# An attention, routed experts and FFN kernel: the opening of the attention reordered, and products of ones in TensorE's waits

## The reference

```python
# q, k, v: (4, 12, 448, 64)
scores = matmul(q, k.T) / sqrt(64) - log(448)
x = matmul(sigmoid(scores), v)            # tokens (1792, 768)

logits = x @ w_gate                       # (1792, 8)
# (token, expert) pairs in falling order of logit; a pair is taken where the
# token is free and the expert has under 224 tokens
out[mask_e] = relu(x[mask_e] @ w1[e]) @ w2[e]      # for the 8 experts e, F = 1024

h = x @ w_in                              # (768, 2048)
out = (max(h, 0) + alpha * min(h, 0)) @ w_out
```

## Time and profile before

| | |
|---|---|
| median of 3 runs | 1068.9 us (1068.49 to 1069.94) |
| profiled execution, its time | 1074.37 us |
| profiled execution, its span | 1072.7 us |
| mean granted clock | 0.964 |
| TensorE busy | 978.1 us, 91% |
| VectorE busy | 588.4 us, 55% |
| ScalarE busy | 393.0 us, 37% |
| HBM traffic | 206 GB/s over the span |

### The profile page before, as it was taken

How to read it: one execution, slowest core, us unless ns; L and a number is a source line. 1 busy time by engine, 2 the same in 40 slices (tenths; PEclk the granted TensorE clock), 3 DMA queues, 4 the chain that set the end, 5 groups by cost and what they waited for, 6 DMA issues and landing times.

```text
span 1072.7 us, 16546 instructions
## 1 busy us (share of the span) xinstructions
PE 978.1 (91%) x6340; PEld 841.6 (78%) x6340; DVE 588.4 (55%) x1454; ACT 393.0 (37%) x628; POOL 185.5 (17%) x202
## 2 busy tenths in 40 slices
PE   5999999806969999799999999999999999999994
PEld 3555555406969898699989998998899999989993
DVE  2344444597765836966954586497539637211110
ACT  4676777401042123346312224542222355122212
POOL 0010110105150010233301014350100325100001
PEclk9999999956979999999999999999999999999997
DMA  9799997317379586847777855679685446966501
GB/s 213 204 260 270 275 264 228 135 35 236 103 206 363 191 221 181 285 128 223 265 280 235 239 177 130 190 222 368 208 241 195 151 129 188 375 231 220 177 1 51
DMA packets 121476, 222.32 MB, mean 207 GB/s; under 512 B 51424, under 2 KB 69216, under 8 KB 121408
## 3 DMA queue, kind: packets, MB, share of 16 engines
q1 hardware_dynamic: 88064, 120.34, 35.7%
q0 software_dynamic: 21280, 91.59, 27.4%
q10 hardware_dynamic: 12064, 9.47, 3.4%
HBM read 184.84 MB, written 36.52 MB: 206 GB/s over the span
## 4 chain that ended last, share of the span: by engine, by line
PE 83%; DVE 10%; ACT 2%; DMA 1%; issue 1%; POOL 0%; SPq 0%; ACTq 0%; DVEq 0%; POOLq 0%
PE psum L886 19%; PE psum L874 19%; PE psum L821 11%; PE psum L851 11%; PE psum L633 7%; PE psum L617 7%; DVE hits L1348 4%; PE psum L816 2%; PE psum L601 2%; PE psum L846 2%; PE psum L644 1%; DVE unit L1243 1%; DMA stage<-x_rows,tok_idx 1%; PE psum L768 1%; PE psum L652 1%
## 5 line engine op out<-in xcount | busy, mean ns | idle before, releaser
L886 PE MATMUL psum<-g_high,unit 128*128 128x448 f32 x768 | 231.7, 369 | 6.4 <-DVE g_low L1271 6.2
L874 PE MATMUL psum<-y_high,unit 128*128 128x448 f32 x768 | 231.5, 369 | 4.6 <-ACT below L1021 4.3
L886 PEld LDWEIGHTS psum<-g_high,unit 128*128 128x128 f32 x768 | 144.3, 188 | 21.8 <-DVE g_low L1271 9.9
L874 PEld LDWEIGHTS psum<-y_high,unit 128*128 128x128 f32 x768 | 144.3, 188 | 18.8 <-ACT below L1021 5.8
L874 PE MATMUL psum<-y_low,unit 128*128 128x448 f32 x384 | 140.5, 366 | 0.0
L886 PE MATMUL psum<-g_low,unit 128*128 128x448 f32 x384 | 140.5, 366 | 0.0
L1243 DVE TENSOR_TENSOR unit<-raw,unit 128x768 fp32r<-128x768 f32 (+1 forms) x106 | 109.3, 1060 | 39.7 <-ACT unit L994 39.2
L1020 ACT ACTIVATE above<-psum 128x448 f32<-128x448 f32 x64 | 35.0, 546 | 246.2 <-PE psum L874 246.2
L821 PE MATMUL psum<-x_high,unit 128*128 128x224 f32 x672 | 119.8, 280 | 2.9 <-DVE unit L1243 2.9
L1266 DVE SCALAR_TENSOR_TENSOR below<-below,neg_alpha,above 128x448 f32<-128x448 f32 x64 | 43.8, 684 | 138.1 <-ACT below L1021 137.7
L851 PE MATMUL psum<-h_high,unit 128*128 128x224 f32 x672 | 117.2, 278 | 2.5 <-issue 2.5
(11 more groups left out here) (159 smaller groups left out, 1278.7 us busy)
## 6 DMA issues: line engine op xcount, KB each, us to landing
unit<-ffn_parts SPq DMA_DIRECT2D x120, 768.0 KB, 6.4
ffn_parts<-pre_parts POOLq DMA_DIRECT2D x24, 768.0 KB, 5.7
ffn_parts<-unit SPq DMA_DIRECT2D x8, 768.0 KB, 5.5
q_in<-in_q_dram SPq DMA_DIRECT2D x24, 224.0 KB, 3.9
k_in<-in_k_dram SPq DMA_DIRECT2D x24, 224.0 KB, 5.9
v_in<-in_v_dram SPq DMA_DIRECT2D x24, 224.0 KB, 6.2
x_rows<-x_tok POOLq DMA_DIRECT2D x8, 672.0 KB, 5.5
rank_in<-suit_flat POOLq DMA_DIRECT2D x6, 896.0 KB, 14.2
```

The costliest lines, as they stand in the source:

```text
L874: last = pe.matmul(psum[:, IN_BANK, 0:PAIR], w, y[:, c, :], start=(c == 0 and i == 0), stop=(c == DC - 1 and i == 2))
L886: last = pe.matmul(psum[:, OUT_BANK + d, 0:PAIR], w, g[:, m % 2, :], start=(m == 0 and i == 0), stop=(m == FC - 1 and i == 2))
```

## The change

The attention's opening:

- ACT issues the first k, ahead of `w_gate` and `alpha`; SP issues the others. In the first batch SP does not wait for the semaphores that VectorE sets, and v of a pair is issued after q and k of the next pair.
- POOL's diagonal pattern has a semaphore of its own; VectorE makes `ones_f` first and `ident` next, before the other patterns. TensorE waits for `ident_done` in place of `const_done`.
- ACT does a Sigmoid of one column of ones into `counts` before it waits for `const_done`.
- TensorE does 12 products of `ones_f` with itself, then `turn_qk(0,0)`, `score(0,0,0)`, `turn_qk(0,1)`, `score(0,0,1)`. ACT does `sigmoids(0,0,0)` before the roundings of pair 1.

The routings: `keep_busy(n, bank)` issues n bf16 products of `ones_b` (112 x 112) with 448 columns of ones, into a PSUM bank that holds nothing. 120 stand after `turn_suit(0)`, 12 after `spread_thr(0)`, 18 after `sum_flags(0)`, and at step `OWN` 22 before and 12 after `turn_first(1)`.

```diff
+    FILLERS = 12
+    BUSY_SEARCH, BUSY_FLAGS, BUSY_PLACES, BUSY_TOKENS, BUSY_SPLIT = 120, 12, 18, 22, 12
...
 # SP
-            with sp.Fori(0, B) as b:
-                for hp in range(PAIRS):
-                    n = pair(b, hp)
-                    sp.wait_ge(qk_turned, turned(n - RING, 1))
-                    sp.dma_start(q_in[hp % RING][:], rows(q)).then_inc(qk_loaded[hp % RING], 16)
-                    sp.dma_start(k_in[hp % RING][:], rows(k)).then_inc(qk_loaded[hp % RING], 16)
-                    sp.wait_ge(heads_done, heads(n - V_RING))
-                    sp.dma_start(v_in[hp % V_RING][:], ...)
+            def load_qk(b, hp, first):
+                n = pair(b, hp)
+                if not first or n >= RING:
+                    sp.wait_ge(qk_turned, turned(n - RING, 1))
+                sp.dma_start(q_in[hp % RING][:], pair_rows(q, b, hp)).then_inc(qk_loaded[hp % RING], 16)
+                if not first or n > 0:
+                    sp.dma_start(k_in[hp % RING][:], pair_rows(k, b, hp)).then_inc(qk_loaded[hp % RING], 16)
+            def load_v(b, hp, first):
+                if not first:
+                    sp.wait_ge(heads_done, heads(pair(b, hp) - V_RING))
+                sp.dma_start(v_in[hp % V_RING][:], ...)
+            def load_batch(b, first):
+                for hp in range(PAIRS + 1):
+                    if hp < PAIRS:
+                        load_qk(b, hp, first)
+                    if hp > 0:
+                        load_v(b, hp - 1, first)
+            load_batch(0, True)
+            with sp.Fori(1, B) as b:
+                load_batch(b, False)
...
 # POOL
-                last.then_inc(iota_done, 1)
+                last.then_inc(diff_done if at == I_DIFF else iota_done, 1)
...
 # TensorE
-            pe.wait_ge(const_done, 1)
+            pe.wait_ge(ones_done, 1)
+            for i in range(FILLERS):
+                pe.matmul(psum[:, i % JT, 0:128], ones_f[:], ones_f[:], start=True, stop=True)
+            pe.wait_ge(ident_done, 2)
             turn_qk(0, 0)
+            score(0, 0, 0)
             turn_qk(0, 1, second=True)
-            score(0, 0, 0)
             score(0, 0, 1)
...
+            def keep_busy(n, bank):
+                for _ in range(n):
+                    pe.matmul(psum[0:P, bank, 0:4 * P], ones_b[:], ones_b[:].unsqueeze(1).to_broadcast([P, 4, P]),
+                              start=True, stop=True)
...
                 if s == OWN:
+                    keep_busy(BUSY_TOKENS, EC // 2 - 1)
                     turn_first(1)
+                    keep_busy(BUSY_SPLIT, EC // 2 - 1)
...
             turn_suit(0)
+            keep_busy(BUSY_SEARCH, Y_BANK)
             spread_thr(0)
+            keep_busy(BUSY_FLAGS, Y_BANK)
             sum_flags(0)
+            keep_busy(BUSY_PLACES, Y_BANK)
             sum_idx(0)
...
 # ACT
+            act.dma_start(k_in[0][:], first_k).then_inc(qk_loaded[0], 16)
             act.dma_start(w_gate_sb[:], w_gate.rearrange("(c p) e -> p c e", p=128)).then_inc(small_loaded, 16)
             act.dma_start(alpha_sb[:], alpha).then_inc(small_loaded, 16)
+            act.wait_ge(ones_done, 1)
+            act.activation(counts[:], ones_f[:, 0:1], ACT.Sigmoid)
             act.wait_ge(const_done, 1)
...
             for hp in range(2):
                 for i in range(2):
                     round_qk(0, hp, i, second=(hp == 1))
-            sigmoids(0, 0, 0)
+                if hp == 0:
+                    sigmoids(0, 0, 0)
...
 # DVE
+            dve.memset(ones_f[:], 1.0).then_inc(ones_done, 1)
...
-            dve.wait_ge(iota_done, len(IOTAS))
+            dve.wait_ge(diff_done, 1)
+            dve.tensor_copy(iota_f[:, I_DIFF:I_DIFF + 128], iota_i[:, I_DIFF:I_DIFF + 128]).then_inc(ident_done, 1)
+            dve.wait_ge(ident_done, 1)
+            dve.tensor_scalar(ident[:], iota_f[:, I_DIFF:I_DIFF + 128], 0.0, None, ALU.is_equal).then_inc(ident_done, 1)
+            dve.wait_ge(iota_done, len(IOTAS) - 1)
...
-            dve.tensor_scalar(ident[:], iota_f[:, I_DIFF:I_DIFF + 128], 0.0, None, ALU.is_equal)
-            dve.memset(ones_f[:], 1.0)
```

More of the change, by code:

```diff
@@ L237, in attention_routed_moe_prelu_ffn @@
         TX = RT[:, 512 - 2 * P:512]
+        ones_done = sem("ones_done")
+        diff_done = sem("diff_done")
+        ident_done = sem("ident_done")
         iota_done = sem("iota_done")
@@ L348, in probs_of, with pair_rows @@
             return PROBS0 + 4 * n + 2 * step + h + 1
+        def pair_rows(src, b, hp):
+            return src[bass.ds(b, 1), 2 * hp:2 * hp + 2].rearrange("a h (p j) d -> p j (a h) d", p=P)
+        first_k = pair_rows(k, 0, 0)
         OWN = DC + EC
@@ L431, in _ @@
         def _(sp):
-            with sp.Fori(0, B) as b:
-                for hp in range(PAIRS):
-                    def rows(src):
-                        return src[bass.ds(b, 1), 2 * hp:2 * hp + 2].rearrange("a h (p j) d -> p j (a h) d", p=P)
-                    n = pair(b, hp)
-                    sp.wait_ge(qk_turned, turned(n - RING, 1))
-                    sp.dma_start(q_in[hp % RING][:], rows(q)).then_inc(qk_loaded[hp % RING], 16)
-                    sp.dma_start(k_in[hp % RING][:], rows(k)).then_inc(qk_loaded[hp % RING], 16)
-                    sp.wait_ge(heads_done, heads(n - V_RING))
-                    sp.dma_start(v_in[hp % V_RING][:],
-                                 v[bass.ds(b, 1), 2 * hp:2 * hp + 2].rearrange("a h (p j) d -> p (a h) j d", p=P)).then_inc(v_loaded[hp % V_RING], 16)
+            def load_qk(b, hp, first):
+                n = pair(b, hp)
+                if not first or n >= RING:
+                    sp.wait_ge(qk_turned, turned(n - RING, 1))
+                sp.dma_start(q_in[hp % RING][:], pair_rows(q, b, hp)).then_inc(qk_loaded[hp % RING], 16)
[4 more added lines that the diff above has]
+                    sp.wait_ge(heads_done, heads(pair(b, hp) - V_RING))
+                sp.dma_start(v_in[hp % V_RING][:],
+                             v[bass.ds(b, 1), 2 * hp:2 * hp + 2].rearrange("a h (p j) d -> p (a h) j d", p=P)).then_inc(v_loaded[hp % V_RING], 16)
+            def load_batch(b, first):
[7 more added lines that the diff above has]
+                load_batch(b, False)
             for piece in range(PRE_ALL - PRE_RING, PRE_ALL):
@@ L1106, in _ @@
             dve.sem_inc(pre_split, PRE0)
-            dve.wait_ge(iota_done, len(IOTAS))
+            dve.wait_ge(diff_done, 1)
[3 more added lines that the diff above has]
+            dve.wait_ge(iota_done, len(IOTAS) - 1)
             for at, n, _, _, _ in IOTAS:
-                last = dve.tensor_copy(iota_f[:, at:at + n], iota_i[:, at:at + n])
+                if at != I_DIFF:
+                    last = dve.tensor_copy(iota_f[:, at:at + n], iota_i[:, at:at + n])
             last.then_inc(const_step, 1)
```

## The result

| | before | after |
|---|---|---|
| median of 16 runs each, same chip | 1070.49 us (1068.17 to 1073.77) | 1064.81 us (1062.98 to 1068.21) |
| profiled execution, its time | 1074.37 us | 1063.21 us |
| profiled execution, its span | 1072.7 us | 1061.5 us |

The ratio is 0.994, 95% interval 0.993 to 0.9951: faster by 5.7 us. I had forecast 1057.9 us in a range of 1054 to 1063.5, so the time lies outside it, and the gain is about half of the 11.0 us. Yet the two profiled executions are 11.2 us apart. Both facts need an explanation.

The account below looks back on a forecast made before the run. TensorE, busy 91% of the span, was taken as the bound, with time only in its waits and low clock. Opening 6.8 + first routing 0.8 + second expert 3.4 = 11.0 us off 1068.9 gave 1057.9 us, range 1054 to 1063.5.

Parts of the forecast that it names:

- steps 1 to 8: Attention's opening, from first q and k to `score(0,1,1)`: start at 21.5 instead of 28.3 us, 6.8 us gained.
- step 1: Opening: q and k issued at 0.9 us, both landed at 4.9; upper bound 6.3, from the second k's 5.40 us.
- the bound of 6.3: Opening: latest landing of the first k, by the 5.40 us of the second k; opening then gives 6.3 us.
- step 3: Opening: 12 products of ones at 0.25 us each, 3.0 us, from 1.1 to 4.1, hidden by q and k landing.
- steps 4 to 7: Opening: transposes at 4.9, ACT's first copy 6.8, `score(0,0,0)` at 8.55, second table load gone, `score(0,1,0)` at 17.7 not 22.54.
- Rival B: Attention is bound by DMA after all and swallows the opening's gain: 1064.7 us; 5 in 100.
- The table load: Opening: ACT's 1.28 us load moves to about 2.4 us, hidden; copy needs no third load; second load gone.
- The search's 120: First routing: 120 products from 212.5 end at 236.7 to 238.6, TensorE needed at 238.56; hidden.
- 12: 2.4 us in the 3.3 free: First routing: the 12 flags products take 2.4 us within 3.3 us free on TensorE, so hidden.
- the term of 0.8 us: First routing: high clock shortens thr, flags and the token sum by 0.3 + 0.1 + 0.4 us.
- Rival D: Products of ones too slow, search block ends some 19 to 23 us late at low level: 1080 us; 3 in 100.
- Do these pass on?: Routings: gains pass on, as queues behind depend on TensorE's progress; second expert's high clock gives 3.4 us in all.

Follow-up runs that it names:

- kernel 7: New opening without its 12 products of ones and with none in the routings, against the kernel before: 1066.52 us, ratio 0.9951.
- kernel 3: The kernel before with only `keep_busy` and its five calls in the routings, on the old opening: 1071.98 us, ratio 1.0008 to the kernel before.
- kernel 5: New opening with only the 22 and 12 products around the second expert's transposes, against the kernel before: 1065.21 us, ratio 0.9935.
- kernels 3 and 4: The second of these: the whole change with 134 search products in place of 120, against the kernel before: 1063.74 us, ratio 0.9931.

## Why the prediction was wrong, by its own steps

Starts of TensorE's work in the profiled executions, in us earlier than in the kernel before:

| start of | changed | opening alone | 22 and 12 | 22 and 12, pass moved |
|---|---|---|---|---|
| `score(0,1,1)` | 8.7 | 8.7 | 8.7 | 8.2 |
| suitability transposes | 8.8 | 8.8 | 8.7 | 8.3 |
| flags' sums | 8.0 | 9.4 | 8.9 | 7.5 |
| first expert's transposes | 8.0 | 9.5 | 9.0 | 7.4 |
| second expert | 8.8 | 8.9 | 10.3 | 7.8 |
| its second half | 11.5 | 8.5 | 13.0 | 10.5 |
| first FFN | 10.1 | 8.5 | 10.7 | 10.5 |
| second expert pair | 10.3 | 8.5 | 9.1 | 10.5 |

In the last profile the suitability transposes ran low (3.23 us for the 16 against 1.75), so its search began later; that is its smaller lead at the flags.

- **The opening, steps 1 to 8: right in mechanism, too small.** 6.8 us forecast, 8.7 us in the profiles, 8.0 us in the medians (1063.2 against 1071.2). Two sizes were off and opposed. In step 1 I took k to be there at 4.9, and wrote that nothing else is in flight; with nothing in its way the transpose waited until 6.18. SP now issues the next pairs without waiting, and of the transfers issued in the first 4 us k took 5.0 us to land in kernel 7 and 5.3 in the changed one, against 4.0 before. That is near the bound of 6.3 that I had kept, and what the rule says that I weighed there and set aside: the Trainium skill (DMA: Bandwidth & Descriptors, Issuing engines are not separate DMA queues) has only the issue time saved. The trace agrees: nothing beyond the issue time was gained, and of its 1.6 us only 0.3, for k was there at 6.18 in kernel 7 and by the old order at 6.5 (2.50 + 4.0). It cost little, since ACT started at 6.95. In step 3 the products of ones were 24 of 0.21 us and I saw in them only a cost; they had the clock up before 6.25, so that steps 4 to 7 ran high as well. Without them, in kernel 7, `score(0,1,0)` starts at 17.68 and `score(0,1,1)` at 21.50, the 17.7 and 21.5 of the forecast. That agreement is in part luck, since the score blocks before them start 0.7 and 0.8 us later than forecast; the 1.9 us between the two kernels are what the products bring.
- **It passes on.** Rival B is wrong: 8.7 us at 20 us are 8.8 us at 201 us.
- **The table load.** One, hidden, and the copy needed none of its own, as forecast. Of a further time beside the load there was no sign: ACT's Sigmoid began at 4.26, 0.02 us after the load's end.
- **The search's 120 was mis-sized.** I priced a product at 0.203 us, from rows of L886, and counted on low products at the start; that put the end at 236.7 to 238.6 (the lower end should read 237.2), at most 1.9 us before the threshold. A product took 0.19 us. The 120 ended 3.4 us early where the clock had stayed high (whole change) and still 2.2 us early where it was low at the start (kernel 3), and both times the clock fell behind them. I had checked whether they would be late and not whether they would be early. What I called hidden, "12: 2.4 us in the 3.3 free", was counted at the high level only (the earlier trace rows have 3.02 free): at the low one they cost 1.4 us at the flags. So the term of 0.8 us came out as a loss of 0.9; with 134 or 128 products the profiles have the 0.7 to 0.8. Rival D had the right mechanism at the wrong place.
- **The step that failed: "Do these pass on?"** I answered it with a sentence and no row, and put 3.4 us on it. The high clock did bring the second expert 2.7 us (11.5 less 8.8) as forecast; VectorE's three passes, behind the last split of the weights, stood before the split of y, and 1.4 us of it went at the first FFN product, 2.3 us in kernel 5, and 2.7 in the routing alone. Where TensorE idles there the clock can fall for some 3.4 us more, which took another 1.7 us in kernel 5 (10.7 to 9.1) and 1.5 in kernels 3 and 4. With one pass moved behind the split of y the same products are worth 2.1 us. The prediction's own last sign of being wrong, a gain at 321 us given back in the first FFN, named the place; the sum gave it no price.
- **The reference of the sum.** I set 11.0 us against the median of three runs, 1068.9; over 86 executions it is 1071.2, and over the 16 beside this result 1070.5. Three executions that spread by 1.5 us say little of a kernel whose executions spread by 7 (1067.7 to 1075.0, and one of 1081.5). This alone moves the forecast by 1.6 to 2.3 us, more than the 1.3 us by which the time lies outside the range. It does not save the mechanism: set against 1071.2, the same sum gives 1060.2, still 4.6 us under what was measured. Those are the routings' 4.2 that never came and, in the medians, 1.6 that their products took away beside, less the 1.2 by which the opening brought more than forecast.
- **A reading.** Slice 11, which I counted into the clock's first dip, reads 9 in the earlier trace rows; the low stretch from 530 to 540 us (mean 0.83) does not show in that line at all.

**What stays open.** The two profiled executions differ by 11.2 us, the medians by 5.7. The profiled one of before lies some 3 us above its median and the one of after 1.6 below its own. Part is where the clock's falls lie: both have 3.4 us at the low level near the fourth expert's second half, which the profile of the opening alone has not. Of the 11.2 us, 10.3 are there at the second expert pair; another 0.8 arise in the third FFN, where the profile of before runs its products slightly slower from 782 to 832 us, with no wait and no fall of the granted clock shown. Why is open. The last weights were issued 10.3 us earlier than before (306.6 against 316.9), and ACT rounded them only 7.6 us earlier (320.4 against 328.0). That the FFN's transfers compete with them was argued from the chain and a full DMA share, and not tried by itself.

## What to carry to other kernels

Work that only keeps the clock up has to end just before the engine is needed. Count it from both sides, with the clock high and low at its start: here 120 products ended 2.2 to 3.4 us early and the clock fell behind them, turning 0.8 us of gain into 0.9 of loss, while 128 and 134 met the need within 0.3 us in the three profiles that have them, all with the clock low at the start. Before counting a gain on one engine as passed on, write down what the in-order engine that it next waits for has in its queue, and how early that work can come; here a single search pass in front of a split hid a gain of 2.1 us altogether. And take the reference from as many executions as the effect needs: a profile is one execution, and three of them may all lie on one side.

## What the runs showed of the hardware

- An f32 product of 128 columns by a full 128 x 128 stationary operand shows as two instructions (24 for 12), 0.21 us each in the changed kernel (24 in 5.12 us). In the ten profiles that have them the 24 took 4.5 to 5.5 us, and the four transposes behind them 0.55 to 0.76 us, against 0.98 without them (kernel 7). A bf16 product of 448 columns took 0.19 us at the high level and 0.39 at the low (12 in 4.71 us).
- The clock fell near 227.7 us after 1.9 us without work (whole change, from 225.8), and at another time held over waits of 1.5 and 1.1 us close together at the start of the FFN (whole change), where it fell after waits of 2.3 to 2.8 us (kernels 3, 4 and 5).
- The last gathered weights of the second expert landed 13.8 us after their issue, while FFN parts of 768 KB each were in flight (11 were issued from 300 to 330 us, 11.2 us from issue to landing in the median).
